# Routing a mixture of experts by ranks within each expert: rows of 18 chunks made early by VectorE and ScalarE

## What is computed

```python
# attention: B, H, S, D = 4, 8, 768, 48; its output is x, 3072 tokens x 384
logits = x @ w_gate + modality_bias[modality_id]      # 3072 x 8
e_idx = argmax(logits)                                # one expert for each token
gate_w = softmax(logits)[e_idx]
for e in range(8):
    h = relu(x[e_idx == e] @ w1[e])                   # 384 x 1024
    out[e_idx == e] = gate_w * (h @ w2[e])            # 1024 x 384
# then: xn = rmsnorm(out) * g; (silu(xn @ w_gate2) * (xn @ w_val)) @ w_out
```

## Time and profile before

| | |
|---|---|
| median of 3 runs | 840.31 us (838.2 to 841.05) |
| the profiled execution | 840.49 us |
| its span in the trace | 838.6 us |
| TensorE busy | 817.1 us, 97% of the span |
| VectorE busy | 337.6 us, 40% |
| ScalarE busy | 297.9 us, 36% |
| GpSimd busy | 149.6 us, 18% |
| mean granted clock of TensorE | 0.992 of full speed |
| last logits to first expert product | 133.07 to 155.26 us |

### The profile page before, as it was taken

One profiled execution on the slowest core, in us unless ns is written; L12 is line 12 of the kernel. 1 busy time (PEld: TensorE's weight loads), 2 busy tenths in 40 slices (PEclk: granted clock), 3 DMA queues, 4 the chain that ended last, 5 costly groups with the idle time before them and its releaser, 6 DMA issues.

```text
span 838.6 us, 14657 instructions
## 1 busy us (share of the span) xinstructions
PE 817.1 (97%) x5247; PEld 744.1 (89%) x5247; DVE 337.6 (40%) x654; ACT 297.9 (36%) x735; POOL 149.6 (18%) x142
## 2 busy tenths in 40 slices
PE   8999996999999999999999999999999999999998
PEld 6888884799999999998889889988988998898888
DVE  6999997832226322314340242034124303411320
ACT  6887784333336333423221222123122202221220
POOL 5987651222212222200000000000000000000000
PEclk9999998899999999999999999999999999999999
DMA  8888842422235232111000100200010010000001
GB/s 260 267 248 249 256 147 104 142 86 101 67 106 183 75 102 76 61 61 41 1 1 29 47 1 11 67 0 0 28 47 0 9 66 0 0 19 19 1 1 38
DMA packets 28784, 63.21 MB, mean 75 GB/s; under 512 B 4530, under 2 KB 17102, under 8 KB 28736
## 3 DMA queue, kind: packets, MB, share of 16 engines
q1 hardware_dynamic: 24224, 52.71, 19.8%
q0 software_dynamic: 3328, 9.45, 3.5%
q10 hardware_dynamic: 1184, 0.45, 0.2%
HBM read 48.83 MB, written 14.56 MB: 76 GB/s over the span
## 4 chain that ended last, share of the span: by engine, by line
PE 81%; DVE 2%; issue 0%; DMA 0%; POOL 0%; ACT 0%; POOLq 0%; DVEq 0%
PE bank L1394 79%; PE bank L1387 1%; PE bank L1451 1%; DVE row_hot L1062 1%; DMA xg<-x_tok,order 0%; POOL xg L618 0%; DVE col_hot L1059 0%; PE bank L1289 0%; DVE xn_lo L1221 0%; DVE xn_hi L1230 0%; DVE xg_lo L1112 0%; DVE place L1049 0%; ACT xg_hi L758 0%; PE bank L1374 0%; ACT o_sb L857 0%
## 5 line engine op out<-in xcount | busy, mean ns | idle before, releaser
L1394 PE MATMUL bank<-xn_hi,ffn_hi 128*128 128x512 f32 x432 | 168.1, 389 | 0.8 <-DVE xn_lo L1221 0.8
L1394 PE MATMUL bank<-xn_hi,ffn_lo 128*128 128x512 f32 x432 | 168.2, 389 | 0.0
L1394 PE MATMUL bank<-xn_lo,ffn_hi 128*128 128x512 f32 x432 | 168.1, 389 | 0.0
L1242 DVE TENSOR_TENSOR prod<-silu,bank 128x512 f32<-128x512 f32 x72 | 49.5, 688 | 286.1 <-ACT silu L845 286.1
L845 ACT ACTIVATE silu<-bank 128x512 f32<-128x512 f32 x72 | 43.1, 598 | 219.5 <-PE bank L1394 219.5
L1394 PE MATMUL bank<-ffn_hi,hh 128*128 128x384 f32 x288 | 97.1, 337 | 0.0
L1394 PEld LDWEIGHTS bank<-xn_hi,ffn_hi 128*128 128x128 f32 x432 | 81.1, 188 | 17.8 <-issue 1.1
L1394 PE MATMUL bank<-ffn_hi,hl 128*128 128x384 f32 x288 | 96.3, 334 | 0.0
L1394 PE MATMUL bank<-ffn_lo,hh 128*128 128x384 f32 x288 | 96.3, 334 | 0.0
L1394 PEld LDWEIGHTS bank<-xn_hi,ffn_lo 128*128 128x128 f32 x432 | 81.1, 188 | 16.9
L1394 PEld LDWEIGHTS bank<-xn_lo,ffn_hi 128*128 128x128 f32 x432 | 81.1, 188 | 16.7
(11 more groups left out here) (195 smaller groups left out, 1277.7 us busy)
## 6 DMA issues: line engine op xcount, KB each, us to landing
rk_in<-rk_t SPq DMA_DIRECT2D x24, 448.0 KB, 4.1
rkn_in<-rk_n SPq DMA_DIRECT2D x24, 384.0 KB, 4.5
ffn_raw<-ffn_w SPq DMA_DIRECT2D x12, 576.0 KB
w_raw<-w SPq DMA_DIRECT2D x16, 384.0 KB, 5.1
y_in<-y_tok SPq DMA_DIRECT2D x6, 770.0 KB, 4.5
v_in<-v_n SPq DMA_DIRECT2D x24, 192.0 KB, 4.0
x_tok<-x_sb SPq DMA_DIRECT2D x24, 192.0 KB, 2.1
out<-o_sb SPq DMA_DIRECT2D x24, 192.0 KB, 1.9
```

The lines of the kernel that those rows point to most:

```text
L1242: v.tensor_tensor(prod[f % 2][:], silu[f % 2][:], ps_v[f % 2], ALU.mult).then_inc(prod_ready, 1)
L1394: last = pe.matmul(dst, left[a], right[b2], start=first and n == 0, stop=end and n == 2)
```

## The change

The place of a token is no longer one number. The rank of a token within its expert gives its row (low 7 bits) and a part of its column (`sub_n`); only the column needs the expert's start, which is now added as a number of columns (`start_n`). Starts are multiples of 256, so rows don't depend on them.

So the rows of the first 18 chunks are made before the last chunk's logits are there. `early_places`, behind sum_logits, multiplies the early ranks by chosen, sums over experts, splits the result and makes 4 of the row_hots. ScalarE makes the other 14, between attention's last xt copy and its last x_sb copy, as the square of row minus column number, and after the x_sb copy turns them into one-hots by one Relu of 1 minus the square over all 14. `early_choice` sums totals within each expert by a scan with a mask (`same_e`, made by two GpSimd memsets at the start). After the counts, VectorE works on the six late chunks' ranks between the steps of the counts, makes start_e and start_n, and six late row_hots in two groups of three. KEEP_CHOICE goes from 8 to 5, and 6 products of 128 columns (KEEP_SPLIT) stand between turn_tile(0) and the first tile. The index products wait for the four, the fourteen and the late groups apart.

```diff
+LATE_HOTS = 2
+FIRST_HOTS = 4
-KEEP_CHOICE = 8
+KEEP_CHOICE = 5
+KEEP_SPLIT = 6
...
+            nc.gpsimd.memset(same_e[:], 1.0).then_inc(same_ready, 1)
+            pool.wait_ge(same_ready, 1)
+            nc.gpsimd.memset(same_e[:, 0:E * EARLY:EARLY], 0.0).then_inc(same_ready, 1)
...
+            one = iota[:, 1:2]
+            far = slice(FIRST_HOTS, EARLY)
+            act.wait_ge(early_rows, 5)
+            for t in range(FIRST_HOTS, EARLY):
+                nc.scalar.activation(row_hot[:, t, :], iota_b[:], ACT.Square, bias=row_f[:, t:t + 1], scale=-1.0).then_inc(far_hots, 1)
             act.wait_ge(lg_ready, B + 1)
             leave_x(NT - 1, (NT - 1) % 2, B, 0)
+            act.wait_ge(far_hots, EARLY - FIRST_HOTS)
+            nc.scalar.activation(row_hot[:, far, :], row_hot[:, far, :], ACT.Relu, bias=one, scale=-1.0).then_inc(far_hots, 1)
...
                     v.memset(upto[:, 0:1], 0.0)
-                    v.tensor_tensor_scan(upto[:, 1:], one, ps_total, 0.0, ALU.mult, ALU.add).then_inc(step, 1)
+                    v.tensor_tensor_scan(upto[:, 1:E * EARLY], ps_total[:, 0:E * EARLY - 1], same_e[:, 1:], 0.0,
+                                         ALU.add, ALU.mult).then_inc(step, 1)
                     dve.wait_ge(step, 6)
-                    v.tensor_tensor(early_n[:], before_late, before[:, :, 0], ALU.subtract)
-                    v.tensor_tensor(place_e[:, :, early], before, rank[:, :, early], ALU.add)
+                    v.tensor_tensor(early_n[:], upto[:, last_of_e], ps_total[:, last_of_e], ALU.add)
+                    v.tensor_tensor(rank_e[:, :, early], before, rank[:, :, early], ALU.add).then_inc(early_rows, 1)
...
+            def early_places():
+                dve.wait_ge(early_rows, 1)
+                v.tensor_tensor(rank_e[:, :, early], rank_e[:, :, early], chosen[:, :, early], ALU.mult).then_inc(early_rows, 1)
+                dve.wait_ge(early_rows, 2)
+                v.tensor_reduce(rank_n[:, early], rank_e[:, :, early].rearrange("p e t -> p t e"), AX_X, ALU.add).then_inc(early_rows, 1)
+                dve.wait_ge(early_rows, 3)
+                v.tensor_copy(rank_i[:, early], rank_n[:, early]).then_inc(early_rows, 1)
+                dve.wait_ge(early_rows, 4)
+                v.tensor_scalar(sub_i[:, early], rank_i[:, early], 7, None, ALU.logical_shift_right)
+                v.tensor_scalar(row_i[:, early], rank_i[:, early], P - 1, None, ALU.bitwise_and).then_inc(step, 1)
+                dve.wait_ge(step, 7)
+                v.tensor_copy(sub_n[:, early], sub_i[:, early])
+                v.tensor_copy(row_f[:, early], row_i[:, early]).then_inc(early_rows, 1)
+                dve.wait_ge(early_rows, 5)
+                dve.wait_ge(marks_ready, 2)
+                for t in range(FIRST_HOTS):
+                    last = make_row(t)
+                last.then_inc(first_hots, 1)
...
             dve.wait_ge(x_ready, NT - 1)
             sum_logits(EARLY, NC - 1)
+            early_places()
             dve.wait_ge(x_ps, NT)
...
             then(v.tensor_tensor(count[:], early_n[:], ps_late, ALU.add))
+            v.tensor_tensor(rank_e[:, :, late], early_n[:].unsqueeze(2).to_broadcast([P, E, NT - EARLY]), rank[:, :, late], ALU.add)
             then(v.tensor_tensor(over[:], ...))
+            v.tensor_tensor(rank_e[:, :, late], rank_e[:, :, late], chosen[:, :, late], ALU.mult)
             then(v.tensor_reduce(tiles[:], over[:], AX_X, ALU.add))
+            v.tensor_reduce(rank_n[:, late], rank_e[:, :, late].rearrange("p e t -> p t e"), AX_X, ALU.add)
             then(v.tensor_tensor_scan(tiles_upto[:], ones_b[:, 0:E], tiles[:], 0.0, ALU.mult, ALU.add))
+            v.tensor_copy(rank_i[:, late], rank_n[:, late])
             v.tensor_scalar(none[:], tiles_upto[:], 0.0, None, ALU.is_le)
-            v.tensor_tensor(place_e[:, :, late], ...)
             then(v.tensor_tensor(start[:], tiles_upto[:], tiles[:], ALU.subtract))
+            v.tensor_scalar(row_i[:, late], rank_i[:, late], P - 1, None, ALU.bitwise_and)
+            v.tensor_scalar(sub_i[:, late], rank_i[:, late], 7, None, ALU.logical_shift_right)
             v.tensor_reduce(expert_f[:], none[:], AX_X, ALU.add)
-            then(v.scalar_tensor_tensor(shift[:], start[:], float(TE), before[:, :, 0], ALU.mult, ALU.subtract))
+            then(v.scalar_tensor_tensor(start_e[:], start[:].unsqueeze(2).to_broadcast([P, E, NT]), float(SUB), chosen[:],
+                                        ALU.mult, ALU.mult))
             v.tensor_copy(expert_0[:], expert_f[:]).then_inc(expert_0_ready, 1)
-            then(v.tensor_tensor(place_e[:], place_e[:], shift[:].unsqueeze(2).to_broadcast([P, E, NT]), ALU.add))
-            then(v.tensor_tensor(place_e[:], place_e[:], chosen[:], ALU.mult))
-            then(v.tensor_reduce(place[:], place_e[:].rearrange("p e t -> p t e"), AX_X, ALU.add))
-            then(v.tensor_copy(place_i[:], place[:]))
-            v.tensor_scalar(col_i[:], place_i[:], 7, None, ALU.logical_shift_right)
-            then(v.tensor_scalar(row_i[:], place_i[:], P - 1, None, ALU.bitwise_and))
-            v.tensor_copy(col_b[:], col_i[:])
-            then(v.tensor_copy(row_f[:], row_i[:]))
+            v.tensor_copy(sub_n[:, late], sub_i[:, late])
+            v.tensor_copy(row_f[:, late], row_i[:, late])
+            then(v.tensor_reduce(start_n[:], start_e[:].rearrange("p e t -> p t e"), AX_X, ALU.add))
+            then(v.tensor_tensor(col_b[:], start_n[:], sub_n[:], ALU.add))
...
-            for t in range(NT):
-                last = v.tensor_scalar(row_hot[:, t, :], iota_b[:], row_f[:, t:t + 1], None, ALU.is_equal)
+            for t in range(EARLY, NT):
+                last = make_row(t)
...
             turn_tile(0)
+            for _ in range(KEEP_SPLIT):
+                pe.matmul(bank[6][:, 0:P], ident, ident, start=True, stop=True)
```

More of the change, by code:

```diff
@@ L61 @@
 NO_TOKEN = 1 << 13
-HOTS = 4
+LATE_HOTS = 2
+FIRST_HOTS = 4
 DN = 2
@@ L166, in build @@
         start = sb("start", [P, E], F32, logits)
[L167 to L171, removed]
+        same_e = sb("same_e", [P, E * EARLY], BF16, logits)
+        rank_e = sb("rank_e", [P, E, NT], F32, logits)
+        start_e = sb("start_e", [P, E, NT], F32, logits)
+        rank_n = sb("rank_n", [P, NT], F32, logits)
+        rank_i = sb("rank_i", [P, NT], I32, logits)
+        start_n = sb("start_n", [P, NT], F32, logits)
+        sub_i = sb("sub_i", [P, NT], I32, logits)
+        sub_n = sb("sub_n", [P, NT], F32, logits)
         row_i = sb("row_i", [P, NT], I32, logits)
@@ L267, in build @@
         hots_ready = sem("hots_ready")
+        early_rows = sem("early_rows")
+        first_hots = sem("first_hots")
+        far_hots = sem("far_hots")
+        same_ready = sem("same_ready")
         ids_ps = sem("ids_ps")
@@ L936, in _ @@
             early, late = slice(0, EARLY), slice(EARLY, NT)
-            one = ones_b[:, 0:1].to_broadcast([P, E * EARLY])
             before = upto[:, 0:E * EARLY].rearrange("p (e t) -> p e t", e=E)
-            before_late = upto[:, EARLY:1 + E * EARLY:EARLY]
+            last_of_e = slice(EARLY - 1, E * EARLY, EARLY)
             rank = ps_rank.rearrange("p (e t) -> p e t", e=E)
@@ L963, in early_choice, with make_row @@
                     dve.wait_ge(ranks_ps, 1)
+                    dve.wait_ge(same_ready, 2)
                     v.memset(upto[:, 0:1], 0.0)
-                    v.tensor_tensor_scan(upto[:, 1:], one, ps_total, 0.0, ALU.mult, ALU.add).then_inc(step, 1)
+                    v.tensor_tensor_scan(upto[:, 1:E * EARLY], ps_total[:, 0:E * EARLY - 1], same_e[:, 1:], 0.0,
+                                         ALU.add, ALU.mult).then_inc(step, 1)
                     dve.wait_ge(step, 6)
-                    v.tensor_tensor(early_n[:], before_late, before[:, :, 0], ALU.subtract)
-                    v.tensor_tensor(place_e[:, :, early], before, rank[:, :, early], ALU.add)
+                    v.tensor_tensor(early_n[:], upto[:, last_of_e], ps_total[:, last_of_e], ALU.add)
+                    v.tensor_tensor(rank_e[:, :, early], before, rank[:, :, early], ALU.add).then_inc(early_rows, 1)
+            def make_row(t):
+                return v.tensor_scalar(row_hot[:, t, :], iota_b[:], row_f[:, t:t + 1], None, ALU.is_equal)
+            def early_places():
[16 more added lines that the diff above has]
+                last.then_inc(first_hots, 1)
             def batch(b):
@@ L1022, in _ @@
             bring_bias(late, NC)
-            dve.wait_ge(step, 7)
+            dve.wait_ge(step, 8)
             find_top(late, NC)
-            dve.wait_ge(step, 8)
+            dve.wait_ge(step, 9)
             mark_top(late, NC)
-            dve.wait_ge(step, 9)
+            dve.wait_ge(step, 10)
             number_top(late, NC)
-            dve.wait_ge(step, 10)
+            dve.wait_ge(step, 11)
             find_best(late, NC)
-            dve.wait_ge(step, 11)
+            dve.wait_ge(step, 12)
@@ L1032, in _ @@
```

(21 more changed lines are left out.)

1 line of the change is left out of this document (removed).

## The result

The change took 834.58 us in the median of 7 runs (833.59 to 835.5), the kernel before 839.15 beside it: a ratio of 0.9941 with a 95% interval of 0.9923 to 0.9958. It is faster by 4.6 us. Two later sets of the change gave 834.47 and 834.46, at ratios of 0.9944 and 0.9947. The profiled execution has a span of 831.8 us.

A forecast was written before the change was run, and what follows sets the result against it. TensorE, busy nearly all the span, bounds the kernel; routing pays only between attention's end and the first expert product. Gains 3.60 + 1.65 - 0.2 = 5.05 us from the median 840.31 give 835.3, stated as 835.4; range 833.9 to 837.8.

The forecast's parts named there:

- likeliest case: Whole kernel: the forecast itself, 835.4 us, own range 834.4 to 836.3, chance 0.60.
- Early rows in the hole: VectorE's 2.50 us rest ending at 133.07, while attention finishes: early steps and four row_hots fit, 2.34 us, free.
- Counts and places: VectorE, chain from count to col_hot: 1.57 us removed, 1.14 added, gain 0.43 (0.0 to 0.7).
- Row_hot: VectorE behind col_hot: six rows, 2.50 us, instead of 24, 5.43; two stalled by GpSimd; gain 2.93 us.
- Index matmuls: Start of tile_n: set by VectorE's three small steps, not TensorE's products, at 143.2; gain of the stretch 3.60 us.
- ScalarE's rows: ScalarE: 14 Squares 4.2 us, Relu about 1.9; w1 loads 1.9 later but hidden by 2 us.
- charge of 0.2: Gather: w1 traffic moves towards the gather's; 0.2 us lost, from 0 to 1.
- The filler and the clock: TensorE before the first product: KEEP_SPLIT fills the idle gap, no clock fall; gain 1.65 us (minus 0.5 to 1.65).
- The first: Rival, first tile: the clock still falls after a 1.5 us rest; gain only 3.6, 836.8 us; chance 0.25.
- The second: Rival, gather and hole: w1 loads take turns with the gather, early steps spill, half the gain lost; 838.5; chance 0.11.
- The third: Rival, ScalarE: Squares hold the last x_sb and w1; slower, 841.5 us at 0.8 each; chance 0.04.

The follow-up runs named there:

- e7_no_hole: The change with VectorE's early steps put behind the last choice instead of in attention's last chunk: 839.76 us, ratio 1.0019 to the kernel before.
- e5_vector_ids: The change with GpSimd's two id_hot instructions moved to VectorE, between col_hot and the six late row_hots: 835.87 us, ratio 0.9955 to the kernel before.
- e4b_more_squares: The change with ScalarE's 14 Squares made twice, before the last x_sb copy: 838.05 us, ratio 0.9986 to the kernel before.
- e2_before_split: The kernel before with only the 12 filler passes (KEEP_SPLIT) added behind the first tile's transposes: 838.93 us, ratio 0.9999 to the kernel before.
- e1_no_split: The change without the 12 filler passes between the first tile's transposes and first product (KEEP_SPLIT 0): 835.52 us, ratio 0.9942 to the kernel before.
- e3_vector_rows: The change with all 18 early row_hots made by VectorE and none by ScalarE: 837.36 us, ratio 0.9972 to the kernel before.
- e6_pair_rows: The change with the six late row_hots made by two tensor-tensor comparisons of three chunks each: 835.47 us, ratio 0.9971 to the kernel before.

## Why the prediction was right, point by point

The forecast was 835.4 us, 5.05 below the median before (840.31); 834.58 was measured, 4.6 below the kernel before beside it (839.15). Its likeliest case is the one that came in the profiled executions. In the number there is some luck: the base, a median of three, was 1.2 too high and the gain 0.5 too large, and the two take each other back in part.

- **Early rows in the hole.** 2.34 with 0.16 to spare forecast; 0.22 to spare found. e7_no_hole shows that the cover was worth 1.6 us at count and 3.0 at the first product.
- **Counts and places.** Gain of 0.43 forecast; from count to col_hot it is 3.42 us now against 3.94, so 0.52. start_e takes 0.35 and costs 0.39 with its gap, as taken. Eight instructions, not nine, are queued between the dependent steps, and they cost about 0.65 where 0.75 was taken.
- **Row_hot.** 2.50 forecast, 2.50 found: two stopped rows and four free ones. e5_vector_ids shows that GpSimd's instructions are what stops them. A price by the mean of 24 rows would have been wrong by 1.1 us.
- **Index matmuls.** tile_n bound by VectorE's own steps, as forecast; the whole stretch gained 3.7 where 3.60 was forecast.
- **ScalarE's rows.** 4.2 and 1.77 us against 4.2 and 1.9. w1 was done 1.6 us before it was wanted, against 2. What I had wrong is what this slack is worth: I let the copies of w1 decide from 2 us later on, and e4b_more_squares and e7_no_hole show that the gather pays first, 1.2 to 1.3 us when the loads run beside it. The charge of 0.2 for the change itself was about right (0 to 0.3).
- **The filler and the clock: the term that came out smaller.** 1.65 us forecast. In the profiled pair it is 1.49: the 72 passes take 8.90 and not 8.7. A median is over executions, though, and the forecast took the profiled one of before for all of them. The routing's 3.6 (22.24 to the first product in the mean of before and e2_before_split, 18.6 in the mean of the change's three) leaves 0.9 of the 4.5 between the medians for the clock, and e1_no_split has the filler at 0.9 to 1.1; neither is clear of the noise by itself. The same filler was worth 0.2 in the kernel before. Why there so little, the runs don't settle. The falls of the clock aren't fixed in place: in the trace of before the 16 filler passes behind the late ranks take 7.10 us and the 14 beside the gather 6.06, in that of e2_before_split 5.41 and 6.69. Most executions of the kernel before have a mean clock below 0.9955 with and without the filler (23 of 26, and 10 of 12), while those of the change do so in 8 of 31. So the shorter pauses of the new order may take falls away that the filler alone doesn't; that is an argument from counts, and it isn't clean: e3_vector_rows has the new order and the filler, but in its trace a pause of 3.9 us instead of 1.9 before the late ranks, and is below 0.9955 in 9 of 10.
- **The rivals.** The first, the clock's fall in the first tile, did not show in any of the change's three profiled executions (72 passes in 8.90 each time), though TensorE rested 1.76 us before the transposes, more than the 1.5 that it names; it shows in the trace without the filler. Its ground, that all falls follow rests of 1.5 us, was too broad: in the trace of before the clock also falls near 145.9, among rests of 0.5 to 0.9 us. The second, giving back half the gain, took twice the Squares or the loss of the hole, and neither exceeded the time before by more than the measurement tells. The third was priced wrongly: with 2 us of slack and 5.05 of gain, all of the gain is gone at 7 us later (Squares at 0.8) and not at 5.5, unless the clock's gain is lost with it. The Squares took 0.30 each, so nothing hung on it.

## What to carry to other kernels

Look for the rest of an engine that a late input causes, and make everything there that doesn't depend on it; then price the work left on the chain by its single instructions, since a mean over 24 hid that two of them stood still for another engine. A store or a copy that is moved behind such work gates whatever its queue does next: follow it to the transfers, and ask what they will meet. A gain read from one profiled execution holds for the median only if the execution is like the others: compare its time and mean clock with theirs first.

## What the runs showed of the hardware

A 128x128 bf16 one-hot on VectorE costs 0.163 us in a row of them (e5_vector_ids: six in 1.06), and 0.98 to 1.03 us while a GpSimd instruction of 1 to 1.25 us runs beside it; a comparison with two inputs in SBUF is stopped as well (e6_pair_rows: 2.61 us for two). ScalarE makes a 128x128 Square in 0.30 us (14 in 4.20). A gather of 256 rows by GpSimd takes 3.1 us from its second issue in the trace of the change, where 1.5 MB of weight loads are issued 5.6 us before it, and 4.25 to 4.40 in e7_no_hole and e4b_more_squares, where they are issued 4.2 and 3.8 us before it. In e4b_more_squares TensorE rested 3.02 us before the transposes; the granted clock was 0.50 (1.2 GHz) from 151 to 154 us, six transposes took 1.52 us instead of 0.85, and twelve filler passes 2.18 instead of 1.50.
